# Strassen's scheme for the first matrix of the second network, in a fused linear-attention kernel

## The chip, the cores and the metric

The kernel runs on one core of a Trainium2 chip. The metric is the device time of one execution in microseconds (us): 1276.09 us for the kernel before, the median of 3 runs (1276.03 to 1276.48).

## What is computed

The reference is a linear attention over 8 batches, 8 heads, 576 positions of 64 values, followed by two feed-forward networks over the 4608 tokens of 512 values. All of it is float32. The change touches the second network:

```
def _moe2_ref(x, w_in, w_out, g_ln):        # x 4608x512, w_in 512x1024, w_out 1024x512
    h = x @ w_in
    h_max = np.max(h, axis=-1, keepdims=True)
    e = np.exp(h - h_max)
    sm = e / (np.sum(e, axis=-1, keepdims=True) + 1e-09)
    solu = h * sm
    mu = np.mean(solu, axis=-1, keepdims=True)
    var = np.mean((solu - mu) ** 2, axis=-1, keepdims=True)
    ln = (solu - mu) / np.sqrt(var + 1e-06) * g_ln
    return (ln @ w_out).astype(np.float32)
```

## The kernel before

TensorE (PE) gets its precision from float32r in two parts: each operand x is held as xh, the value rounded by a copy to float32r, and xl = x - xh. A product of two such operands is three matmuls: high by high, high by low, low by high. Each line of matmuls below is such a triple, each matmul 128 rows deep with 512 columns.

The work has two stages. In the **first stage**, nine chunks of 512 tokens go through attention and the first network (`up` into bank pairs `ps_h`, the activation on VectorE and ScalarE, `down` into `ps_y`). A chunk's result goes to DRAM (`y_scratch`) by `y_copy` on ScalarE and `store_y` on SyncE (SP). In chunk 8, `LAST`, the weights of the second network are loaded and split as well. In the **second stage** 36 tiles of 128 tokens go through the second network, four tiles r = 0..3 for each m = 0..8. For one tile:

- `m1_product` (L1315, matmuls L1328, L1329, L1333): 4 parts of the depth of 512 by 2 halves of 1024 columns by 3 matmuls, 24 in all, into one of two bank pairs, `ps_m` for even tiles and `ps_h` for odd ones.
- `softmax_tile` on VectorE (DVE): the maximum (L1104, reads the banks), sum and reciprocal (L1113, L1115), the product `solu` = h x 1/sum x e (L1117, reads the banks and `e2`), the mean (L1120).
- ScalarE (ACT): `exp_tile` (L776, reads the banks), `square_tile` (L783, sums the squares).
- `norm_tile`: the variance on DVE (L1126), the power -1/2 on GpSimd (POOL, L609), then `z` on DVE (L1132), a transpose in blocks of 32 by 32 on DVE (L1138) into `zb`.
- SP stores `zb` to DRAM (`store_z`, L449) and loads it back in four pieces with the blocks in transposed places (`load_z`, L455); ACT and DVE split it into `zh` (L795) and `zl` (L1142).
- `m2_product` (L1402 to L1404): 24 matmuls into `ps_y`; ACT copies the result (L805) and SP stores it (L442).
- The next x tiles are loaded (`load_x2`, L430), copied to their high part on ACT (L811), and the low part is made on POOL (L575).

Every engine has its order written out by hand and runs it strictly in that order; semaphores are the waits. On PE the order is first product of tile r+1, second product of tile r-2:

```
            def tiles(m, first=False, last=False):
                for r in range(4):
                    if not (first and r == 0 or last and r == 3):
                        m1_product(m + (r + 1) // 4, (r + 1) % 4, first=(first and r < 3))
                    if r >= 2:
                        m2_product(m, r - 2, first=first)
                    elif not first:
                        m2_product(m - 1, r + 2)
```

## Time and profile before

| | |
|---|---|
| median of 3 runs | 1276.09 us |
| the profiled execution's own time | 1276.15 us |
| its span in the profile | 1274.3 us |
| PE busy | 1260.3 us, 99% of the span |
| DVE, ACT, POOL busy | 709.6, 387.3, 346.2 us |
| PE's granted clock | 0.997 of full speed |

The span is the time between the first and the last instruction of the profile. Busy is the time in which at least one instruction of that engine ran; a matmul's record is longer than the distance to the next one, since matmuls overlap in the array. So the price of one matmul is read from the distance of two starts, not from its record. Stage two begins at about 875 us.

### The profile page before, as it was taken

Reading aid. Unit: us, or ns where it says so; the run is one execution under the profiler, and the core shown is the slowest. Engines: PE = TensorE matmul, PEld = TensorE weight load, DVE = VectorE, ACT = ScalarE, POOL = GpSimd, SP = SyncE. Lnnn points to the kernel's source line nnn. Section 1 sums busy time; section 2 is a strip of 40 time slices with the busy share of each in tenths; the row PEclk is TensorE's granted clock in tenths of the full one; section 3 lists DMA queues with packets and bytes.
Section 4 is the critical chain, followed back from the end, with each engine's and each line's share of the span. In section 5 each row is a group of like instructions: output and inputs, shape, how many; then the busy total and the mean of one; then the engine's idle time right before and its main releaser. Section 6 shows DMA issues by size and latency. Waiting matters only on the chain.

```text
span 1274.3 us, 16844 instructions
## 1 busy us (share of the span) xinstructions
PE 1260.3 (99%) x6181; PEld 1035.7 (81%) x6181; DVE 709.6 (56%) x989; ACT 387.3 (30%) x625; POOL 346.2 (27%) x289
## 2 busy tenths in 40 slices
PE   7999999999999999999999999999999999999998
PEld 6788887887887887887887888888888888888887
DVE  7865645645645745645745323346755555555553
ACT  4333212212212212212222212124544444444432
POOL 5333233233233233233233222223111111111110
PEclk8999999999999999999999999999999999999999
DMA  8532313313313313313312101210644444444432
GB/s 207 141 120 70 101 38 113 98 37 111 99 37 110 100 37 108 102 37 108 103 37 70 67 1 69 64 67 29 206 155 147 148 142 138 148 147 141 148 124 75
DMA packets 151569, 127.41 MB, mean 100 GB/s; under 512 B 58584, under 2 KB 131824, under 8 KB 150640
## 3 DMA queue, kind: packets, MB, share of 16 engines
q1 hardware_dynamic: 151488, 126.96, 33.0%
q8 instruction: 20, 0.33, 0.1%
q14 instruction: 13, 0.11, 0.0%
q10 hardware_dynamic: 48, 0.01, 0.0%
HBM read 82.33 MB, written 44.61 MB: 100 GB/s over the span
## 4 chain that ended last, share of the span: by engine, by line
PE 97%; DVE 2%; ACT 0%; issue 0%; DMA 0%; POOL 0%; DVEq 0%
PE ps_h L1262 10%; PE ps_h L1264 10%; PE ps_h L1263 10%; PE ps_y L1278 10%; PE ps_y L1279 10%; PE ps_y L1280 10%; PE ps_y L1403 5%; PE ps_y L1404 5%; PE ps_y L1402 5%; PE ps_m L1329 3%; PE ps_h L1329 3%; PE ps_h L1333 3%; PE ps_m L1333 3%; PE ps_h L1328 3%; PE ps_m L1328 3%; PE ps_m L1188 2%
## 5 line engine op out<-in xcount | busy, mean ns | idle before, releaser
L560 POOL TENSOR_TENSOR gl<-tg,gh 128x512 fp32r<-128x512 f32 x144 | 192.7, 1338 | 580.3 <-ACT gh L686 580.3
L686 ACT ACTIVATE gh<-tg 128x512 fp32r<-128x512 f32 x144 | 91.0, 632 | 592.7 <-PE ps_y L1280 427.5
L998 DVE TENSOR_SCALAR tg<-ps_h,acols 128x512 f32<-128x512 f32 x144 | 107.7, 748 | 235.5 <-PE ps_h L1264 233.7
L1262 PE MATMUL ps_h<-xh,W 128*128 128x512 f32 x576 | 227.2, 394 | 0.1
L1264 PE MATMUL ps_h<-xh,W 128*128 128x512 f32 x576 | 224.8, 390 | 0.0
L1263 PE MATMUL ps_h<-xl,W 128*128 128x512 f32 x576 | 224.6, 390 | 0.0
L1278 PE MATMUL ps_y<-gh,WO 128*128 128x512 f32 x576 | 224.6, 390 | 0.0
L1279 PE MATMUL ps_y<-gl,WO 128*128 128x512 f32 x576 | 224.5, 390 | 0.0
L1280 PE MATMUL ps_y<-gh,WO 128*128 128x512 f32 x576 | 224.5, 390 | 0.0
L1262 PEld LDWEIGHTS ps_h<-xh,W 128*128 128x128 f32 x576 | 108.2, 188 | 23.7 <-DVE W L989 0.5
L1264 PEld LDWEIGHTS ps_h<-xh,W 128*128 128x128 f32 x576 | 108.2, 188 | 22.8
L1280 PEld LDWEIGHTS ps_y<-gh,WO 128*128 128x128 f32 x576 | 108.2, 188 | 22.5
L1279 PEld LDWEIGHTS ps_y<-gl,WO 128*128 128x128 f32 x576 | 108.2, 188 | 22.4
L1278 PEld LDWEIGHTS ps_y<-gh,WO 128*128 128x128 f32 x576 | 108.2, 188 | 22.4
L1263 PEld LDWEIGHTS ps_h<-xl,W 128*128 128x128 f32 x576 | 108.3, 188 | 21.7
L1402 PE MATMUL ps_y<-WO,zh 128*128 128x512 f32 x288 | 112.3, 390 | 0.0
L1404 PE MATMUL ps_y<-WO,zl 128*128 128x512 f32 x288 | 112.2, 390 | 0.0
L1403 PE MATMUL ps_y<-WO,zh 128*128 128x512 f32 x288 | 112.2, 390 | 0.0
L1001 DVE SCALAR_TENSOR_TENSOR tg<-ps_h,tg 128x512 f32<-128x512 f32 x144 | 99.6, 692 | 5.0
L1402 PEld LDWEIGHTS ps_y<-WO,zh 128*128 128x128 f32 x288 | 54.1, 188 | 11.2
L1404 PEld LDWEIGHTS ps_y<-WO,zl 128*128 128x128 f32 x288 | 54.1, 188 | 11.1
L1403 PEld LDWEIGHTS ps_y<-WO,zh 128*128 128x128 f32 x288 | 54.1, 188 | 11.1
(166 smaller groups left out, 1633.5 us busy)
## 6 DMA issues: line engine op xcount, KB each, us to landing
z_scratch<-zb SPq DMA_DIRECT2D x35, 512.0 KB, 2.6
zt<-z_scratch SPq DMA_DIRECT2D x140, 128.0 KB, 3.0
y_scratch<-stage SPq DMA_DIRECT2D x36, 256.0 KB, 3.7
A<-k_dram SPq DMA_DIRECT2D x16, 512.0 KB, 4.9
V<-v_dram SPq DMA_DIRECT2D x32, 256.0 KB, 4.7
out_dram<-ost SPq DMA_DIRECT2D x32, 256.0 KB, 2.3
A<-q_dram SPq DMA_DIRECT2D x14, 512.0 KB, 4.9
stage<-kx_scratch SPq DMA_DIRECT2D x6, 1024.0 KB, 4.4
```

The costliest lines, as they stand in the source:

```text
L560: nc.gpsimd.tensor_tensor(gl[:, f % 2, :], tg[:, f % 2, :], gh[:, f % 2, :].bitcast(F32), ALU.subtract).then_inc(gl_ok, 1)
L998: nc.vector.tensor_scalar(tg[:, f % 2, :], ps_h[:, f % 2, :], 0.0, slope[:, f:f + 1], ALU.min, ALU.mult).then_inc(t_ok, 1)
L1001: nc.vector.scalar_tensor_tensor(tg[:, f % 2, :], ps_h[:, f % 2, :], 0.0, tg[:, f % 2, :], ALU.max, ALU.add).then_inc(g_ok, 1)
L1262: nc.tensor.matmul(o, W1[:, f, 0, a, :], xh[:, a, :], start=(a == 0), stop=False)
L1263: nc.tensor.matmul(o, W1[:, f, 0, a, :], xl[:, a, :], start=False, stop=False)
L1264: mm = nc.tensor.matmul(o, W1[:, f, 1, a, :], xh[:, a, :], start=False, stop=(a == KT - 1))
L1278: nc.tensor.matmul(o, WO[:, f, 0, cols], gh[:, f % 2, :], start=(f == 0), stop=False)
L1279: nc.tensor.matmul(o, WO[:, f, 0, cols], gl[:, f % 2, :], start=False, stop=False)
L1280: mm = nc.tensor.matmul(o, WO[:, f, 1, cols], gh[:, f % 2, :], start=False, stop=(f == NF - 1))
L1402: nc.tensor.matmul(o, zh[:, r % 2, f * P:(f + 1) * P], WO2[:, f, 0, :], start=(f == 0), stop=False)
L1403: nc.tensor.matmul(o, zh[:, r % 2, f * P:(f + 1) * P], WO2[:, f, 1, :], start=False, stop=False)
L1404: mm = nc.tensor.matmul(o, zl[:, r % 2, f * P:(f + 1) * P], WO2[:, f, 0, :], start=False, stop=(f == NF2 - 1))
```

## The change

Two tiles of 128 tokens, a **pair**, now go through the first matrix together. A pair is i = 2m + h, 18 of them. The 256 tokens by 512 by 1024 product is cut into two by two blocks and done by seven block products in place of eight (Strassen's scheme, in Winograd's form with few sums). A block product is 2 parts of the depth by 3 matmuls, so 6 matmuls.

- The seven combinations of the weight's blocks are made once, in chunk 8 (`w2_turn` on POOL, `w2_high` on ACT, `w2_low` on DVE). For x, POOL makes four sums of 128x256 a pair (`x2_sums`), ACT copies 128x1024 and 128x768 (`x2_high`), and POOL makes two low parts of these sizes (`x2_low`).
- The seven products go into three banks, `ba` and `bb` (the two of `ps_m`) and `bd` (one of `ps_h`). Block 0 into `ba` is copied out to `p1` by ACT before block 3 adds to the same bank; sums `u1` (before block 4) and `q1` (before block 5) are made by DVE from a bank and `p1`; `c22` is read before block 6. The results c11, c12, c21, c22 are written to `solu` in SBUF, by one ACT copy and three DVE sums. The maximum, `exp` and the product `solu` then read SBUF, no longer the banks.
- `z` moves from DVE to ACT (`norm_tile`, an Identity with scale and bias); its bias is made by a tiny DVE product (`norm_shift`). The variance is a sum scaled by constants, whose factor goes into the gains.
- On PE the order is: seven blocks of pair i, second product of tile 1 of pair i-2, second product of tile 0 of pair i-1. At the start, the blocks of pair 0 stand inside chunk 8 (behind `up` of f = 14), and pair 1 is followed by one second product only. At the end both tiles of pair 17 are transposed by PE (8 transposes each, before: one tile).
- SP's order is, for a pair: output of tile 0 of pair i-2, `store_z` of tile 1 of pair i-1, `load_z` of both tiles of pair i-1, x of pair i+2, output of tile 1 of pair i-2, `store_z` of tile 0 of pair i.

The diff, cut to its core:

```
--- before.py
+++ after.py
-            W2 = sb("W2", [P, 2, KT, F2], F32R)
+            W2c = sb("W2c", [P, 7, 2, 2, TOK], F32R)
             WO2 = sb("WO2", [P, NF2, 2, DM], F32R)
+            solu = sb("solu", [P, 2, F2])
             e2 = sb("e2", [P, 2, F2])
-            solu = sb("solu", [P, 2, F2])
-            junk = sb("junk", [P, F2])
-            z = sb("z", [P, F2])
+            z = sb("z", [P, 2, F2])
             zh = sb("zh", [P, 2, F2], F32R)
             zl = sb("zl", [P, 2, F2], F32R)
-            ost = sb("ost", [P, 2, DM])
...
+            x2raw = sb("x2raw", [P, 2, 2 * TOK])
...
+            xsum = sb("xsum", [P, 3 * 2 * P])
...
+        w2_block = [raw2[a][:, :].rearrange("p (a n) -> p a n", a=2)[:, :, n * TOK:(n + 1) * TOK]
+                    for a in range(2) for n in range(2)]
+        B11, B12, B21, B22 = w2_block
+        w2_part = (B11, B12, B12, B21, B11, B22, B21)
...
+        WO_ORDER = (2, 3, 0, 4, 5, 6, 7, 1)
+        LEFT = (0, 4, 5, 1, 2, 6, 3)
+        p1 = kmax[:, :]
+        u1 = x2b[:, :, :].rearrange("p a n -> p (a n)")
+        q1 = kmt[:, :]
...
+            def pair(m, h, count=2, last=False):
+                before, two_before = ((m - 1, 2), (m - 1, 0)) if h == 0 else ((m, 0), (m - 1, 2))
+                if count >= 2:
+                    store_out(*two_before)
+                if count >= 1:
...
+                    store_z(before[0], before[1] + 1)
...
+                    for t in range(2):
+                        load_z(before[0], before[1] + t)
...
+                if not last:
+                    load_x2(m + 1, h)
+                if count >= 2:
+                    store_out(two_before[0], two_before[1] + 1)
+                if not (last and h == 1):
+                    store_z(m, 2 * h)
...
+            def x2_sums(i, h, m):
+                pool.wait_ge(x2_in[h], 32 * (m + 1))
+                a11, a12, a21, a22 = (x2raw[:, h, n * 2 * P:(n + 1) * 2 * P] for n in range(4))
+                s1, s2, s4 = (xsum[:, n * 2 * P:(n + 1) * 2 * P] for n in range(3))
+                if not (isinstance(i, int) and i == 0):
+                    pool.wait_ge(x2l_ok, 2 * i)
+                nc.gpsimd.tensor_tensor(s1, a21, a22, ALU.add).then_inc(xs_ok, 1)
+                pool.wait_ge(xs_ok, 4 * i + 1)
+                nc.gpsimd.tensor_tensor(s2, s1, a11, ALU.subtract).then_inc(xs_ok, 1)
+                nc.gpsimd.tensor_tensor(a21, a11, a21, ALU.subtract).then_inc(xs_ok, 1)
+                pool.wait_ge(xs_ok, 4 * i + 2)
+                nc.gpsimd.tensor_tensor(s4, a12, s2, ALU.subtract).then_inc(xs_ok, 1)
+            def x2_low(i, h, part):
+                x2h, x2l = x2_parts(i)
+                lo, hi = ((0, 8 * P), (8 * P, 14 * P))[part]
+                src = x2raw[:, h, :] if part == 0 else xsum[:, :]
+                pool.wait_ge(x2h_ok, 2 * i + part + 1)
+                nc.gpsimd.tensor_tensor(x2l[:, lo:hi], src, x2h[:, lo:hi].bitcast(F32),
                                         ALU.subtract).then_inc(x2l_ok, 1)
+            def power(i, t):
+                pool.wait_ge(var_ok, 2 * i + t + 1)
+                nc.gpsimd.tensor_tensor(st[:, t, 8:9], st[:, t, 9:10], mhalf[:, :], ALU.pow).then_inc(rstd_ok, 1)
...
+            for t in range(2):
+                x2_low(1, 1, t)
+            for t in range(2):
+                power(0, t)
+            def pair(m, h, last=False):
+                i = 2 * m + h
+                if not last:
+                    x2_sums(i + 1, 1 - h, m + h)
+                for t in range(2):
+                    if not last:
+                        x2_low(i + 1, 1 - h, t)
+                    power(i, t)
...
+            def p1_copy(i):
+                act.wait_ge(prod, 7 * i + 1)
+                if not (isinstance(i, int) and i == 0):
+                    act.wait_ge(c21_ok, i)
+                nc.scalar.activation(p1, ba, ACT.Copy).then_inc(p1_ok, 1)
+            def c11_copy(i):
+                act.wait_ge(prod, 7 * i + 4)
+                if isinstance(i, int) and i == 0:
+                    act.wait_ge(y_used, NF * LAST + 8)
+                else:
+                    act.wait_ge(z_ok, 2 * i - 1)
+                nc.scalar.activation(solu[:, 0, 0:TOK], ba, ACT.Copy).then_inc(c11_ok, 1)
...
+            def exp_tile(i, t):
+                act.wait_ge(nmax_ok, 2 * i + t + 1)
+                if isinstance(i, int) and i == 0:
+                    act.wait_ge(prod, 7)
+                nc.scalar.activation(e2[:, t, :], solu[:, t, :], ACT.Exp,
+                                     bias=st[:, t, 0:1], accum_out=st[:, t, 1:2]).then_inc(exp_ok, 1)
...
+            def square_tile(i, t):
+                act.wait_ge(nmu_ok, 2 * i + t + 1)
+                if not (isinstance(i, int) and i == 0):
+                    act.wait_ge(zb_ok, 2 * i + t - 1)
+                nc.scalar.activation(z[:, t, :], solu[:, t, :], ACT.Square, bias=st[:, t, 5:6],
+                                     accum_out=st[:, t, 6:7]).then_inc(sq_ok, 1)
+            def norm_tile(i, t):
+                act.wait_ge(nb_ok, 2 * i + t + 1)
+                nc.scalar.activation(z[:, t, :], solu[:, t, :], ACT.Identity, bias=st[:, t, 7:8],
+                                     scale=st[:, t, 8:9]).then_inc(z_ok, 1)
...
+            p1_copy(0)
+            wo2_high(WO_ORDER[2])
+            c11_copy(0)
+            exp_tile(0, 0)
+            x2_high(1, 1)
+            g_high(LAST, NF - 1)
+            exp_tile(0, 1)
+            for f in WO_ORDER[3:]:
+                wo2_high(f)
+            for t in range(2):
+                square_tile(0, t)
+                norm_tile(0, t)
+            y_copy(LAST)
+            def pair(m, h, count=2, last=False):
+                i = 2 * m + h
+                if count >= 2:
+                    out_copy(i - 2, 0)
+                p1_copy(i)
+                c11_copy(i)
+                zt_high(i - 1, 0)
+                exp_tile(i, 0)
+                if not (last and h == 1):
+                    x2_high(i + 1, 1 - h)
+                exp_tile(i, 1)
+                square_tile(i, 0)
+                norm_tile(i, 0)
+                square_tile(i, 1)
+                zt_high(i - 1, 1)
+                norm_tile(i, 1)
+                if count >= 2:
+                    out_copy(i - 2, 1)
...
+            def q1_sum(i):
+                dve.wait_ge(prod, 7 * i + 2)
+                dve.wait_ge(p1_ok, i + 1)
...
+                nc.vector.tensor_tensor(q1, bb, p1, ALU.add).then_inc(q1_ok, 1)
+            def u1_sum(i):
+                dve.wait_ge(prod, 7 * i + 3)
...
+                nc.vector.tensor_tensor(u1, bd, p1, ALU.add).then_inc(u1_ok, 1)
...
+                nc.vector.tensor_tensor(solu[:, 1, TOK:F2], bd, q1, ALU.add).then_inc(c22_ok, 1)
...
+                nc.vector.tensor_tensor(solu[:, 0, TOK:F2], bb, u1, ALU.add).then_inc(c12_ok, 1)
...
+                nc.vector.tensor_tensor(solu[:, 1, 0:TOK], bd, p1, ALU.add).then_inc(c21_ok, 1)
...
+                nc.vector.tensor_reduce(st[:, t, 0:1], solu[:, t, :], AX_X, ALU.max, negate=True).then_inc(nmax_ok, 1)
...
+                nc.vector.scalar_tensor_tensor(solu[:, t, :], solu[:, t, :], st[:, t, 3:4], e2[:, t, :], ALU.mult,
+                                               ALU.mult, accum_out=st[:, t, 4:5]).then_inc(solu_ok, 1)
...
+            def norm_shift(i, t):
+                n = 2 * i + t + 1
+                dve.wait_ge(rstd_ok, n)
+                nc.vector.tensor_tensor(st[:, t, 7:8], st[:, t, 5:6], st[:, t, 8:9], ALU.mult).then_inc(nb_ok, 1)
...
+            def pair(m, h, count=2, last=False):
+                i = 2 * m + h
+                q1_sum(i)
+                u1_sum(i)
+                c22_sum(i)
+                c12_sum(i)
+                max_tile(i, 0)
+                c21_sum(i)
+                max_tile(i, 1)
+                zt_low(i - 1, 0)
+                solu_tile(i, 0)
+                solu_tile(i, 1)
+                norm_stats(i, 0)
+                norm_shift(i, 0)
+                norm_stats(i, 1)
+                zt_low(i - 1, 1)
+                norm_shift(i, 1)
+                if not (last and h == 1):
+                    z_turn(i, 0)
+                    z_turn(i, 1)
...
+                def block(k, bank, more=False):
+                    a = LEFT[k] * 2 * P
+                    if k == 1:
+                        pe.wait_ge(x2l_ok, 2 * i + 2)
+                    if first:
+                        pe.wait_ge(w2_lo, k + 1)
+                    for j in range(2):
+                        hi, lo = (t[:, a + j * P:a + (j + 1) * P] for t in (x2h, x2l))
+                        nc.tensor.matmul(bank, hi, W2c[:, k, 0, j, :], start=(j == 0 and not more), stop=False,
+                                         skip_group_check=more)
+                        nc.tensor.matmul(bank, hi, W2c[:, k, 1, j, :], start=False, stop=False, skip_group_check=more)
+                        mm = nc.tensor.matmul(bank, lo, W2c[:, k, 0, j, :], start=False, stop=(j == 1), skip_group_check=more)
+                    mm.then_inc(prod, 1)
+                if not first:
+                    pe.wait_ge(c11_ok, i)
+                block(0, ba)
+                if not first:
+                    pe.wait_ge(c12_ok, i)
+                block(1, bb)
+                if not first:
+                    pe.wait_ge(c21_ok, i)
+                block(2, bd)
+                pe.wait_ge(p1_ok, i + 1)
+                block(3, ba, more=True)
+                pe.wait_ge(u1_ok, i + 1)
+                block(4, bd, more=True)
+                pe.wait_ge(q1_ok, i + 1)
+                block(5, bb, more=True)
+                pe.wait_ge(c22_ok, i + 1)
+                block(6, bd, more=True)
...
+            def pair(m, h, count=2):
+                i = 2 * m + h
+                m1_pair(i)
+                if count >= 2:
+                    m2_product(i - 2, 1)
+                m2_product(i - 1, 0)
...
+            z_transpose(2 * LAST + 1, 0)
+            m2_product(2 * LAST, 1, turn=True)
+            for t in range(2):
+                m2_product(2 * LAST + 1, t)
```

Where the rows of the order stand now. POOL, for one pair, the last in which x is prepared (`xsum` and `x2raw` hold the sums and the raw x, `st` the statistics). Before, for two tiles:

```order
L575 TENSOR_TENSOR qTl<-V,qTh 128x512 [waits x2h_ok]
L609 TENSOR_TENSOR st<-st,mhalf 128x1 [waits var_ok]
L575 TENSOR_TENSOR qTl<-A,qTh 128x512 [waits x2h_ok]
L609 TENSOR_TENSOR st<-st,mhalf 128x1 [waits var_ok]
L575 TENSOR_TENSOR qTl<-kmax,qTh 128x512 [waits x2h_ok]
```

Now, for one pair:

```order
L608 TENSOR_TENSOR xsum<-x2raw 128x256 [waits x2l_ok,x2_in1]
L610 TENSOR_TENSOR xsum<-xsum,x2raw 128x256 [waits xs_ok]
L611 TENSOR_TENSOR x2raw<-x2raw 128x256
L613 TENSOR_TENSOR xsum<-x2raw,xsum 128x256 [waits xs_ok]
L620 TENSOR_TENSOR xl<-x2raw,xh 128x1024 [waits x2h_ok]
L625 TENSOR_TENSOR st<-st,mhalf 128x1 [waits var_ok]
L620 TENSOR_TENSOR xl<-xsum,xh 128x768 [waits x2h_ok]
```

The second low part stands directly behind the power of tile 0. The power of tile 1 follows it, and the sums for the next pair stand directly behind that one.

DVE, from `solu` to the end of a tile. Before (the `z` row is the one that goes to ACT):

```order
L1142 TENSOR_TENSOR zl<-zt,zh 128x1024 [waits zh_ok]
L1113 TENSOR_SCALAR st<-st 128x1 [waits exp_ok]
L1115 RECIPROCAL st<-st 128x1 [waits se_ok]
L1117 SCALAR_TENSOR_TENSOR solu,st<-ps_h,st,e 128x1024 [waits rs_ok]
L1120 TENSOR_SCALAR st<-st 128x1 [waits solu_ok]
L1126 TENSOR_SCALAR st<-st 128x1 [waits sq_ok]
L1132 TENSOR_SCALAR z<-solu,st 128x1024 [waits zb_ok,rstd_ok]
L1138 STREAM_TRANSPOSE zb<-z 128x1024 [waits zb_st,z_ok]
```

Now, for the two tiles of a pair, behind the maxima and the low part of tile 0 of the pair before:

```order
L1279 RECIPROCAL st<-st 128x1 [waits se_ok]
L1281 SCALAR_TENSOR_TENSOR solu,st<-solu,st,e 128x1024 [waits rs_ok]
L1284 TENSOR_SCALAR st<-st 128x1 [waits solu_ok]
L1277 TENSOR_SCALAR st<-st 128x1 [waits exp_ok]
L1279 RECIPROCAL st<-st 128x1 [waits se_ok]
L1281 SCALAR_TENSOR_TENSOR solu,st<-solu,st,e 128x1024 [waits rs_ok]
L1284 TENSOR_SCALAR st<-st 128x1 [waits solu_ok]
L1289 TENSOR_SCALAR st<-st 128x1 [waits sq_ok]
L1294 TENSOR_TENSOR st<-st 128x1 [waits rstd_ok]
L1289 TENSOR_SCALAR st<-st 128x1 [waits sq_ok]
L1308 TENSOR_TENSOR zl<-A,zh 128x1024 [waits m2_done,zh_ok]
L1294 TENSOR_TENSOR st<-st 128x1 [waits rstd_ok]
```

L1281 reads `solu` and `e`, both in SBUF, where L1117 read a bank and `e`. L1294 is the new tiny product (`norm_shift`), and the low part of tile 1 of the pair before stands ahead of its second instance. Both transposes follow.

ACT, for one pair (`tg` is the output buffer, `kmax` is `p1`, `A` is `zt`):

```order
L898 ACTIVATE tg<-ps_y 128x512 [waits o_st0,m2_done]
L850 ACTIVATE kmax<-ps_m 128x512 [waits c21_ok,prod]
L858 ACTIVATE solu<-ps_m 128x512 [waits z_ok,prod]
L889 ACTIVATE zh<-A 128x1024 [waits m2_done,zt_in0]
L864 ACTIVATE e,st<-solu,st 128x1024 [waits nmax_ok]
L912 ACTIVATE xh<-x2raw 128x1024 [waits prod,xs_ok]
L912 ACTIVATE xh<-xsum 128x768
L864 ACTIVATE e,st<-solu,st 128x1024 [waits nmax_ok]
L871 ACTIVATE z,st<-solu,st 128x1024 [waits zb_ok,nmu_ok]
L876 ACTIVATE z<-solu,st 128x1024 [waits nb_ok]
L871 ACTIVATE z,st<-solu,st 128x1024 [waits zb_ok,nmu_ok]
L889 ACTIVATE zh<-A 128x1024 [waits m2_done,zt_in1]
```

Behind them come `z` of tile 1 (L876) and the output of tile 1 of pair i-2, and then the next pair's L898 and L850. The copy to `p1` (L850), for which PE waits, thus stands behind all of the pair before.

## Rows read from the trace of the kernel before

**Rows 1.** The page: busy time, and the chain that ended last, by engine.

```profile
PE 1260.3 (99%) x6181; PEld 1035.7 (81%) x6181; DVE 709.6 (56%) x989; ACT 387.3 (30%) x625; POOL 346.2 (27%) x289
...
PE 97%; DVE 2%; ACT 0%; issue 0%; DMA 0%; POOL 0%; DVEq 0%
```

**Rows 2.** Waits of PE: what it waited for, total, times, longest.

```profile
PE ps_m L1163 <- DVE kmax L883: 3.1, 2, 1.7
```

**Rows 3.** Timeline of PE in stage two: start, length, instruction.

```profile
1062.59 0.39 PE L1402 MATMUL ps_y<-WO,zh 128*128 128x512 f32 x1
...
1068.03 0.39 PE L1328 MATMUL ps_h<-W,qTh 128*128 128x512 f32 x1
```

**Rows 4.** Instructions by line and form: busy us, mean ns, idle before.

```profile
L560 POOL TENSOR_TENSOR gl<-tg,gh 128x512 fp32r<-128x512 f32 x144 | 192.7, 1338 | 580.3 <-ACT gh L686 580.3
...
L1142 DVE TENSOR_TENSOR zl<-zt,zh 128x1024 fp32r<-128x1024 f32 x35 | 42.5, 1215 | 0.0
L783 ACT ACTIVATE junk<-solu,st 128x1024 f32<-128x1024 f32 x36 | 41.5, 1153 | 51.2 <-DVE st L1120 51.2
L795 ACT ACTIVATE zh<-zt 128x1024 fp32r<-128x1024 f32 x35 | 37.0, 1057 | 6.6 <-DMA zt<-z_scratch 6.4
...
L1117 DVE SCALAR_TENSOR_TENSOR solu<-ps_m,st,e 128x1024 f32<-128x1024 f32 x18 | 23.1, 1284 | 0.6
...
L1104 DVE TENSOR_REDUCE st<-ps_m 128x1 f32<-128x1024 f32 x18 | 22.0, 1220 | 34.1 <-PE ps_m L1333 34.1
...
L805 ACT ACTIVATE ost<-ps_y 128x512 f32<-128x512 f32 x36 | 21.5, 599 | 15.9 <-PE ps_y L1404 12.9 <-ACT junk L783 1.1
...
L985 DVE TENSOR_TENSOR xl<-ps_m,xh 128x512 fp32r<-128x512 f32 x28 | 19.4, 692 | 45.4 <-ACT xh L675 45.4
```

**Rows 5.** Timeline of one tile in stage two, all engines.

```profile
1062.79 1.22 DVE L1104 TENSOR_REDUCE st<-ps_m 128x1 f32<-128x1024 f32 x1 [2.20 <-PE ps_m L1333]
...
1064.05 1.12 ACT L776 ACTIVATE e<-ps_m,st 128x1024 f32<-128x1024 f32 x1 [4.83 <-DVE st L1104]
...
1065.15 0.62 ACT L811 ACTIVATE qTh<-kmax 128x512 fp32r<-128x512 f32 x1
...
1068.70 0.55 POOL L609 TENSOR_TENSOR st<-st,mhalf 128x1 f32<-128x1 f32 x1 [1.55 <-DVE st L1126]
```

**Rows 6.** Timeline: the way of the first tile's z through DRAM.

```profile
887.73 0.34 SPq L449 DMA_DIRECT2D z_scratch<-zb  x1
890.39 1.75 SPq L455 DMA_DIRECT2D zt<-z_scratch  x4
...
894.94 1.06 ACT L795 ACTIVATE zh<-zt 128x1024 fp32r<-128x1024 f32 x1 [1.23 <-DMA zt<-z_scratch]
```

**Rows 7.** Timeline: DVE beside POOL, in chunk 8 and behind it.

```profile
856.84 1.29 POOL L560 TENSOR_TENSOR gl<-tg,gh 128x512 fp32r<-128x512 f32 x1 [4.15 <-ACT gh L686]
857.41 1.26 DVE L1084 SCALAR_TENSOR_TENSOR WO<-V,acols,WO 128x512 fp32r<-128x512 f32 x1 [2.25 <-ACT WO L818]
...
880.94 0.75 DVE L1084 SCALAR_TENSOR_TENSOR WO<-A,acols,WO 128x512 fp32r<-128x512 f32 x1 [1.88 <-ACT WO L818]
881.51 1.34 POOL L575 TENSOR_TENSOR qTl<-V,qTh 128x512 fp32r<-128x512 f32 x1 [6.60 <-ACT qTh L811]
...
881.99 1.28 DVE L1117 SCALAR_TENSOR_TENSOR solu<-ps_m,st,e 128x1024 f32<-128x1024 f32 x1
```

**Rows 8.** The same at the start of the kernel, POOL's row and DVE's.

```profile
10.82 1.04 POOL L538 TENSOR_TENSOR qTh<-ident,km 128x512 fp32r<-128x512 f32 x1 [8.13 <-DVE km L906]
...
10.91 0.97 DVE L911 TENSOR_TENSOR kml<-km,kmh 128x4 f32<-128x4 f32 x1
```

**Rows 9.** Stretches: busy time of PE, PEld, DVE, ACT, POOL, clock, DMA.

```profile
9.00:12.00 3.00, 0.74 (x5) 0.51 (x5) 2.90 (x7) 0.00 (x0) 1.08 (x2) 0.88 1.31 262
12.00:15.00 3.00, 2.66 (x9) 2.06 (x10) 3.00 (x4) 0.87 (x2) 3.00 (x3) 0.50 1.37 217
...
18.00:21.00 3.00, 3.00 (x63) 2.54 (x64) 2.71 (x5) 2.30 (x3) 2.37 (x2) 0.99 0.28 87
```

560 lines of the change are left out of this document (289 added, 271 removed).

## The prediction

> **What bounds the kernel now.** The page comes first: PE is busy 99% of the span and is 97% of the chain that ended last [rows 1]. The list of PE's waits is next: its largest entry is 3.1 us at the start of the kernel, and nothing in it belongs to stage two [rows 2]. So in stage two PE streams without a gap, and every other engine has slack. The price of a matmul comes from the distance of starts: the 24 matmuls of one second product run from 1062.59 to 1068.03, which is 5.44 us, or 0.2267 us each [rows 3]. Two tiles take 96 matmuls, 21.76 us. The groups by line then give the price of each step on the other engines [rows 4], and the timeline of one tile gives their order and the hand-over times [rows 5]. These steps form a long chain (maximum, exponential, solu, square, power, z, transpose, DRAM, split), but today PE has a first and a second product between any two of its uses, so the chain is never seen.
>
> **Fewer matmuls.** A pair has 7 x 6 = 42 matmuls in place of 48. 18 pairs save 108, and 108 x 0.2267 = 24.5 us. All of it lies on PE, which sets the end. A pair now asks 42 + 48 = 90 matmuls of PE, 20.40 us.
>
> **The new loop.** This gain holds only if PE need not wait. Before, PE's only conditions in stage two were results a tile old or older. Now block 3 waits for `p1`, a copy of block 0 of the same pair. That copy stands on ACT behind all of the pair before, down to its last `z` and two output copies; and that pair's chain starts at its own blocks 3 to 5, which it needs for c12. So the time from one block 3 to the next is at least the length of this loop. I add it up with the rows' durations; an ACT instruction directly behind another costs about 0.1 less than its record (1064.05 to 1065.15 for a record of 1.12), and a hand-over costs 0.04 (the maximum ends at 1064.01, ACT starts at 1064.05) [rows 5].
>
> - Blocks 3, 4, 5: 18 matmuls, 4.08; until DVE starts 0.20 (PE's next product starts at 1062.59, DVE at 1062.79) [rows 3, 5]. At 4.28.
> - c12, a sum of a bank and SBUF, as L985: 0.73. Maximum over 1024, as L1104: 1.25 [rows 4]. At 6.26.
> - The exponential stands on ACT behind `zh` of the pair before, which waits for DRAM. From the issue of the store to that of the load are 2.66, from there to the start of `zh` 4.55 [rows 6]. The store of tile 0 stands on SP behind the output of tile 1 of an older pair, and goes at 24.4 of the loop before; `zh` starts at 6.6 of this one and takes 0.96, so the exponential waits to 7.53.
> - Exponential 1.15; x's high parts, 1024 and 768 wide, 0.96 + 0.71 (1.05 for 1024, 0.62 for 512 [rows 4, 5]); second exponential 1.28; two tiny ones 0.36. At 11.98.
> - `solu` of tile 1: 1.29 as L1117, and 0.84 held up by POOL (below). Mean and variance 0.34, hand-over 0.08, power 0.55 [rows 5]. At 15.1.
> - `norm_shift` 0.19, and 1.60 held up by POOL. `z` on ACT: I take the square's 1.15, less 0.1, as it has the same width and also a bias [rows 4]. At 17.9.
> - Square of tile 1 1.15, `zh` of tile 1 1.09, `zl` 1.22 and 0.33 held up, `norm_shift` 0.10 and 0.50 held up, `z` 1.10. At 23.4.
> - Two output copies 0.51 each and the copy to `p1` 0.64 (L805 [rows 4]). At 25.0.
>
> 25.0 against 20.4 of PE work leaves PE idle for 4.6 us in each pair. What is late next is block 1 of the next pair, for its second low part, by under 0.1. Pair 2 starts from a disturbed order and I take 5 for it, 5.2 for pair 3, 13 x 4.6 = 60 for pairs 4 to 16, and 3.8 for pair 17, behind which POOL has less work. Together 74 us.
>
> **The port.** The largest new term is where POOL holds DVE up. A DVE instruction with two inputs in SBUF took 1.26 us when it started 0.57 behind a POOL one, and 0.75 with POOL idle; the one that reads a bank and SBUF took 1.28 beside POOL, its usual time [rows 7, 4]. Size does not help: a product of 128x4 that started 0.09 behind a POOL instruction of 1.04 ended with it, after 0.97 [rows 8]. `solu` moves from the harmless kind to the other, and `norm_shift` is of that kind. POOL has four sums (0.73 each), two low parts (2.41 and 1.85) and two powers in each pair, estimated from L560's 1.29 at 512 wide and a slope of 2.2 ns per column. Its second low part starts directly behind the power, the very instruction `norm_shift` waits for, so it holds that one up for 1.6 in every pair. These hold-ups are 0.84 + 1.60 + 0.33 + 0.50 = 3.3 us of the loop. Bounds: 0 if DVE always got there first, 4.3 if the first `solu` met the first low part too.
>
> At `norm_shift` the two starts lie within 0.1 us, and a tie could also go DVE's way (third rival). The Trainium skill (SBUF — State Buffer, "Who interferes with whom") has this as a rule against such a change: two SBUF inputs of DVE and a reading GpSimd instruction share one read interface, and the second to issue blocks until the first is done, whatever its size. By it the sum is the forecast's; without it, the second rival's.
>
> **The start of stage two.** In chunk 8 DVE is 1.3 late for the sum before block 4 of pair 0. From the end of pair 0's blocks, PE has 48 matmuls of chunk 8 and three blocks of pair 1, 15.0 us. ACT has in front of `p1` of pair 1: two exponentials, x's high parts, a `g_high`, five copies of weights, both squares and both `z`, and then the four copies of `y_copy`. The squares and `z` wait for DVE, whose five low parts of weights meet POOL's 2.41 and 1.85. Followed in this way it comes to 25.5 us, so 10.1 is wait, and 0.4 is for a low part of x. The first second product then waits 3.8 for its z from DRAM, and pair 2 1.1 for x. Together 16.7 us. Bounds: 10, if DVE and POOL don't meet, and 20.
>
> **The end.** Pair 17 is short of cover: the second product of pair 16 waits for the output copy that stands behind the last `z`, 2.9, and there are 8 more transposes, 0.9. Together 3.8.
>
> **Work with no price.** The seven weight combinations (14 instructions of DVE and ACT, four of POOL) lie in chunk 8, where PE has 24 matmuls, 5.44 us, for each step f, and POOL one L560 [rows 3, 4]. If that cover were gone, they would cost about 1.2 each on DVE (L1142's width). The x loads are two transfers per pair, two pairs ahead. SP's queue is charged above, with the store and the load.
>
> **The sum.** 1276.15 - 24.5 + 74 + 16.7 + 3.8 = 1346.2 us, from the profiled execution's own time, which is 0.06 above the median. My forecast is **1346 us**, slower.
>
> **Rivals.**
> 1. **The clock falls in PE's gaps: 1370 us.** From 9 to 12 us PE was busy for only 0.74, the clock granted was 0.88 in that stretch and 0.50, the lower of the two levels (1.2 GHz), behind it, and 0.99 again from 18 on [rows 9]. A gap of 4.6 in each pair is of that size. At half speed for 2 to 5 us a pair loses 1 to 2.5; 16 pairs at 1.5 are 24 us. Against it: PE works 20 us between two gaps here. The Trainium skill (TensorE: Matmul & The Clock Gate, "Why this matters for your kernels") warns of idle gaps between bursts of matmuls, and by it the fall would come.
> 2. **The loop without the port: 1296 us.** If hand-overs fall so that POOL never holds DVE, the loop is 25.0 - 3.3 = 21.7, idle 1.3 in 16 pairs, 21 us; start 13, end 3, and 7 for DRAM traffic in bursts (two stores and two outputs go out together now). 1276 - 24.5 + 44 = 1296.
> 3. **Only `norm_shift` gets through: 1316 us.** Loop 23.1, idle 2.7, 43 us; start and end 18; traffic 3: 1276 - 24.5 + 64 = 1316. For it: the power's result and the low part's start are under 0.1 apart.
> 4. **Faster, 1262 us.** The loop is shorter than PE's 20.4 us: without the port, and the DRAM way at least 1.3 shorter than now, as one transfer is no longer behind another. Then only the start is paid: 1276 - 24.5 + 10. Its point is a loop of 20.4; by the rows the loop without port and DRAM is still 20.4 to 20.6.
>
> That the change does not do what it says can be left out: the 108 matmuls are gone from the order.
>
> **How the numbers follow.** Forecast 0.42, clock 0.20, third rival 0.15, loop without the port 0.11, faster 0.08, no change 0.04. A measurement of this kernel tells 0.2% (2.6 us) from no change. The forecast's own range is 1332 to 1358: 0.8 either way per pair. The whole range runs from 1292, which takes in the rival without the port, to 1386, the clock falling in nearly every pair; about 0.18 lies outside. Faster 0.08, same 0.04, slower 0.88.
>
> **What would show it.** Right: PE waits for ACT's copy to `p1` 17 times, some 4.6 us each and once about 10; starts of block 0 are 25 us apart; `norm_shift` has a median near 1.7 us for a 128x1 product, and `solu` of one of two tiles lies over 2 us; stage-two PE busy near 82%. Wrong: `norm_shift` at 0.15 (third rival); `solu` at 1.3 too (second); a granted clock under 0.95 behind the gaps (first); PE without waits for `p1` (fourth).

## The result, and the profile after

The changed kernel takes **1386.8 us**, the median of 4 runs (1386.1 to 1388.0), against 1276.08 for the kernel before: a ratio of 1.0867, 95% interval 1.0854 to 1.0881. It is slower, as forecast, but by 110.7 us where 70 were forecast, and 0.8 us above the top of the range. The page of the profile after opens with these rows (busy time of each engine, and the chain that ended last by engine and by line):

```profile
PE 1273.9 (92%) x6081; PEld 1035.7 (75%) x6081; DVE 813.5 (59%) x1084; ACT 459.3 (33%) x700; POOL 453.4 (33%) x363
...
issue 15%; POOL 6%; DVE 5%; PE 4%; ACT 4%; DMA 3%; SPq 0%; POOLq 0%; ACTq 0%; DVEq 0%
POOL xl L620 4%; DVE st L1294 2%; DMA A<-z_scratch 1%; DMA z_scratch<-V 1%; DVE solu L1281 1%; ACT z L871 1%; POOL xsum L610 1%; POOL st L625 1%; ACT zh L889 1%; PE ps_m L1533 1%; ACT e L864 1%; DVE WO L1214 1%; PE ps_m L1536 0%; PE ps_m L1535 0%; ACT xh L912 0%
```

PE was 97% of this chain before [rows 1]; now a mixture of every engine stands there, with POOL's low parts (`xl`, L620) as its first line. (The shares add up to 37%, as the chain is followed back only to about 870 us; "issue" is time in which the profile shows no wait.) PE's waits name the place (what PE waited for, us in total, times, the longest):

```profile
PE ps_m L1533 <- ACT kmax L850: 87.7, 17, 9.1
PE ps_y L1630 <- DVE zl L1308: 3.7, 1, 3.7
...
PE ps_y L1630 <- ACT tg L898: 2.9, 1, 2.9
```

L850 is the copy to `p1` (its buffer is called `kmax`). It is waited for 17 times, 87.7 us in all, one of them 9.1 at the start: the wait that was forecast, where it was forecast, and nearly as long (84 us in the forecast). Nothing of the kind stood in the list before [rows 2].

One wait, in the timeline of PE (start, duration, engine, line, output and inputs, form, idle time before and its releaser):

```profile
1062.64 0.39 PE L1536 MATMUL ps_h<-W2c,xl 128*128 128x512 f32 x1
1068.15 0.80 PE L1533 MATMUL ps_m<-W2c,xh 128*128 128x512 f32 x1 [5.12 <-ACT kmax L850]
1068.74 0.63 PE L1535 MATMUL ps_m<-W2c,xh 128*128 128x512 f32 x1
1069.17 0.63 PE L1536 MATMUL ps_m<-W2c,xl 128*128 128x512 f32 x1
1069.60 0.63 PE L1533 MATMUL ps_m<-W2c,xh 128*128 128x512 f32 x1
...
1072.07 0.39 PE L1535 MATMUL ps_h<-W2c,xh 128*128 128x512 f32 x1
1072.30 0.39 PE L1536 MATMUL ps_h<-W2c,xl 128*128 128x512 f32 x1
```

After 5.1 us of idling the matmuls start 0.427 us apart, twice the 0.227 of [rows 3], and only from about 1071.6 on 0.227 again. The next block 3 starts at 1095.33, so a pair takes 27.18 us here. The other engines' timeline in the same pair:

```profile
1075.67 1.06 ACT L889 ACTIVATE zh<-A 128x1024 fp32r<-128x1024 f32 x1 [3.87 <-DMA A<-z_scratch]
1076.63 1.14 ACT L864 ACTIVATE e<-solu,st 128x1024 f32<-128x1024 f32 x1
...
1079.38 3.05 DVE L1281 SCALAR_TENSOR_TENSOR solu<-solu,st,e 128x1024 f32<-128x1024 f32 x1
1082.96 1.29 DVE L1281 SCALAR_TENSOR_TENSOR solu<-solu,st,e 128x1024 f32<-128x1024 f32 x1
1085.16 1.78 DVE L1294 TENSOR_TENSOR st<-st 128x1 f32<-128x1 f32 x1 [0.66 <-POOL st L625]
...
1078.89 2.46 POOL L620 TENSOR_TENSOR xl<-x2raw,xh 128x1024 fp32r<-128x1024 f32 x1 [12.16 <-ACT xh L912]
1085.10 1.84 POOL L620 TENSOR_TENSOR xl<-xsum,xh 128x768 fp32r<-128x768 f32 x1
```

The `solu` of tile 0 starts 0.49 behind POOL's first low part and takes 3.05; that of tile 1, with POOL idle, takes 1.29. `norm_shift` (L1294), one number a row, takes 1.78 and ends with POOL's second low part.

### The profile page after: what moved, and what is told of

It reads as the page before. It is cut to its first block and busy times, and to the rows that moved or that the text cites. A ratio compares the mean times of both kernels' runs of the same rounds, so it can differ in the third digit from the quotient of the medians.

```text
span 1385.0 us, 17034 instructions
## 1 busy us (share of the span) xinstructions
PE 1273.9 (92%) x6081; PEld 1035.7 (75%) x6081; DVE 813.5 (59%) x1084; ACT 459.3 (33%) x700; POOL 453.4 (33%) x363
## 5 line engine op out<-in xcount | busy, mean ns | idle before, releaser
L1533 PE MATMUL ps_m<-W2c,xh 128*128 128x512 f32 x136 | 63.1, 464 | 88.4 <-ACT kmax L850 87.7
L1467 PEld LDWEIGHTS ps_h<-xh,W 128*128 128x128 f32 x576 | 108.1, 188 | 23.8 <-DVE W L1111 0.5
L1483 PEld LDWEIGHTS ps_y<-gh,WO 128*128 128x128 f32 x576 | 108.1, 188 | 22.9 <-POOL gl L589 0.4
L1469 PEld LDWEIGHTS ps_h<-xh,W 128*128 128x128 f32 x576 | 108.1, 188 | 22.8
L620 POOL TENSOR_TENSOR xl<-x2raw,xh 128x1024 fp32r<-128x1024 f32 x17 | 45.3, 2665 | 196.4 <-ACT xh L912 196.4
L1533 PEld LDWEIGHTS ps_m<-W2c,xh 128*128 128x128 f32 x136 | 29.0, 214 | 101.9 <-ACT kmax L850 94.8
```

The costliest lines, as they stand in the source:

```text
L1467: nc.tensor.matmul(o, W1[:, f, 0, a, :], xh[:, a, :], start=(a == 0), stop=False)
L1469: mm = nc.tensor.matmul(o, W1[:, f, 1, a, :], xh[:, a, :], start=False, stop=(a == KT - 1))
L1483: nc.tensor.matmul(o, WO[:, f, 0, cols], gh[:, f % 2, :], start=(f == 0), stop=False)
L1533: nc.tensor.matmul(bank, hi, W2c[:, k, 0, j, :], start=(j == 0 and not more), stop=False, skip_group_check=more)
```

## The experiments

Three causes are to be told apart: **the port** (POOL's large instructions hold DVE up), **the clock** (it falls in PE's gaps), and **the order** (what ACT's order puts in a row makes the loop, and places POOL's work against DVE's). "Period" below is the distance of two copies to `p1` (or of two c11 copies), averaged over 11 to 13 pairs in the middle of stage two; for the change it is 27.4 us. Ratios are to the kernel before, with 95% intervals.

| kernel | us | ratio | period |
|---|---|---|---|
| the change | 1386.8 | 1.0867 [1.0854, 1.0881] | 27.4 |
| a1 norm_shift, one tensor input | 1348.0 | 1.0567 [1.0550, 1.0585] | 24.3 |
| a2 12 filling matmuls | 1384.0 | 1.0846 [1.0828, 1.0864] | 27.2 |
| b3 20 filling matmuls | 1365.4 | 1.0693 [1.0675, 1.0710] | 25.9 |
| a3 a1 and 12 filling matmuls | 1334.6 | 1.0462 [1.0444, 1.0479] | 23.8 |
| a4 POOL's work 8 columns wide | 1315.8 | 1.0308 [1.0291, 1.0326] | 22.8 |
| b1 z back on VectorE | 1320.2 | 1.0346 [1.0328, 1.0363] | 23.9 |
| c3 ACT's order, first half | 1383.9 | 1.0841 [1.0824, 1.0858] | 27.3 |
| c2 ACT's order, second half | 1363.0 | 1.0677 [1.0661, 1.0694] | 25.9 |
| b2 ACT's order, both halves | 1287.7 | 1.0086 [1.0070, 1.0103] | 21.3 |
| b4 b2 and a1 | 1278.0 | 1.0012 [1.0002, 1.0021] | 20.7 |
| c4 b1 and b2 | 1295.1 | 1.0150 [1.0135, 1.0166] | 22.1 |
| c1 b4 and another start | 1270.3 | 0.9956 [0.9943, 0.9970] | 20.7 |

**a1: one operand of `norm_shift` in another form.**

```
-                nc.vector.tensor_tensor(st[:, t, 7:8], st[:, t, 5:6], st[:, t, 8:9], ALU.mult)
+                nc.vector.tensor_scalar(st[:, t, 7:8], st[:, t, 5:6], st[:, t, 8:9], None, ALU.mult)
```

> One instruction in another form: norm_shift takes the power's result as its per-partition scalar and no longer as a second tensor, so it has one tensor input in SBUF; the number is the same. Theory A (POOL's second low part holds norm_shift up, 1.6 to 1.8 us for tile 1 and 0.5 for tile 0 in each pair, both on the loop from block 3 to block 3): norm_shift falls from 1.78 to about 0.15, the period from 27.2 to about 24.4 us, the time to about 1336 us. Rival B (norm_shift is long because POOL's power hands its result over late, whatever the form): it stays at 1.7 and the time at 1387. Rival C (the length of the order alone, with the DRAM way as its longest piece, sets the period): norm_shift is short, the time goes down by under 10 us.

Measured: 1348.0 us (1343.9 to 1350.1), period 24.3. (In the expectation the tiles are swapped: it is tile 0's `norm_shift` that takes 1.78, tile 1's takes 0.67.) Groups by line of DVE from 940 to 1240 us (busy us, mean ns of one, idle before), the change first and then a1:

```profile
L1281 DVE SCALAR_TENSOR_TENSOR solu<-solu,st,e 128x1024 f32<-128x1024 f32 x22 | 47.6, 2166 | 0.8
L1308 DVE TENSOR_TENSOR zl<-A,zh 128x1024 fp32r<-128x1024 f32 x22 | 31.0, 1409 | 8.8 <-ACT zh L889 8.8
L1294 DVE TENSOR_TENSOR st<-st 128x1 f32<-128x1 f32 x22 | 27.1, 1231 | 7.3 <-POOL st L625 7.3
```

```profile
L1281 DVE SCALAR_TENSOR_TENSOR solu<-solu,st,e 128x1024 f32<-128x1024 f32 x26 | 46.6, 1791 | 0.9
...
L1294 DVE TENSOR_SCALAR st<-st 128x1 f32<-128x1 f32 x24 | 5.0, 208 | 7.9 <-POOL st L625 7.9
```

The same product of 128x1, at the same place and behind the same power, takes 0.21 us in place of 1.23 on average. All that changed is how the second operand is given, so it was not the power's result that came late (rival B falls). The form of a product of one number a row is worth 39 us; a part of that lies in `solu`, whose mean also fell, from 2.17 to 1.79, as the starts on DVE and POOL moved.

The time is still 12 us above the 1336 expected. PE's gaps are now 2.2 to 3.3 us long, and behind 7 of the 16 the clock falls again (spacing 0.43), as at 1056.70, behind a gap of 2.9. Behind the other 9 it does not, though one of them is the longest of all:

```profile
1129.78 0.50 PE L1533 MATMUL ps_m<-W2c,xh 128*128 128x512 f32 x1 [3.29 <-ACT kmax L850]
1130.11 0.39 PE L1535 MATMUL ps_m<-W2c,xh 128*128 128x512 f32 x1
1130.34 0.40 PE L1536 MATMUL ps_m<-W2c,xl 128*128 128x512 f32 x1
```

A pair with a fall takes 25.0 to 26.5 us, one without 23.6 to 24.2, so seven falls cost some 13 us, about what is missing. (This is the execution of 1343.9 us; the other three have a lower clock and take longer.)

**a2 and b3: filling matmuls in PE's gap.** They write a bank that nothing reads.

```
                 block(2, bd)
+                for _ in range(0 if first else 12):
+                    nc.tensor.matmul(ps_h[:, 1, :], x2h[:, 0:P], W2c[:, 0, 0, 0, :], start=True, stop=True)
                 pe.wait_ge(p1_ok, i + 1)
```

> 12 matmuls of 512 columns that write an unused bank stand on PE between block 2 and the wait for p1, in pairs 1 to 17; they bring PE's granted clock through the gap and compute nothing that is read. Theory A (in the gap of 5.1 us the clock falls, and the first blocks behind it run at half speed for 1.6 us): the period goes from 27.2 to about 25.6, the time to 1355 to 1362 us, and the spacing behind the wait stays 0.227. Rival B (the fall is hidden, as the loop waits for DVE and ACT anyway): within 3 us of 1387. Rival C (the filling delays the real blocks): slower than 1387 by up to 10.

> 20 filling matmuls (4.5 us) in place of 12 between block 2 and the wait for p1. With 12 a gap of 2.4 us was left in each pair, and the clock fell behind it all the same. Theory A (a fall costs about 1.6 us a pair, and it comes with gaps of over 2 us, not with those under 1): no spacing over 0.23 us behind the wait, period 25.8, time 1360 to 1364. Rival B (the clock is no term of the loop): 1384 as with 12. Rival C (the filling delays block 3): slower than 1384.

Measured: 1384.0 with 12, only 3 us less; 1365.4 with 20, 21.5 us less. The timeline of PE with 12, then (in the second fence) the only gap with 20 from 1056 to 1084 us:

```profile
1064.41 0.79 PE L1533 MATMUL ps_m<-W2c,xh 128*128 128x512 f32 x1 [2.39 <-ACT kmax L850]
1065.00 0.63 PE L1535 MATMUL ps_m<-W2c,xh 128*128 128x512 f32 x1
1065.43 0.63 PE L1536 MATMUL ps_m<-W2c,xl 128*128 128x512 f32 x1
```

```profile
1063.28 0.50 PE L1533 MATMUL ps_m<-W2c,xh 128*128 128x512 f32 x1 [0.73 <-ACT kmax L850]
```

And the stretch from 925 to 1250 us (length, busy us of PE, PEld, DVE, ACT, POOL with counts, granted clock, DMA share, GB/s), of the change, with 12 and with 20:

```profile
925.00:1250.00 325.00, 265.40 (x1068) 213.90 (x1067) 222.34 (x300) 151.58 (x212) 109.49 (x96) 0.92 0.40 115
```

```profile
925.00:1250.00 325.00, 298.16 (x1235) 240.76 (x1234) 221.09 (x301) 154.40 (x217) 112.10 (x97) 0.95 0.40 115
```

```profile
925.00:1250.00 325.00, 317.09 (x1381) 257.54 (x1380) 220.86 (x310) 157.63 (x223) 119.89 (x101) 1.00 0.42 122
```

My expectation for 12 was wrong: I took it that a gap of about 2.4 us would leave the clock alone, and behind 12 gaps of 2.3 to 2.6 us in a row it fell to the lower level (behind the two before them, of 2.07 and 2.63, it did not). With 20, the gap is 0.7, the clock stays at 1.00, and the period goes down by 1.5 us, the price of the slow first blocks: (0.427 - 0.227) x 8 = 1.6. The clock is a term of the loop of its own, worth 21.5 us, and the filling cost nothing that shows.

**a3: both.** 

> Both edits, norm_shift with one tensor input and the 12 filling matmuls. If port and clock are separate terms, their gains add up but for the shorter gap, which leaves the clock less to lose: about 1324 us, period 23.7. If the two are one and the same cause (the gap is only long because of the port), it is the time of the first edit alone, 1336.

Measured: 1334.6, against 1324 expected. The number alone would fit the rival's 1336, but that was the time expected of a1, and a1 took 1348.0: the filling gives 13.4 us on top of it, where it gave 3 without a1. So the two are separate terms. The granted clock is 1.00 and the waits for `p1` are down to 10.2 us in all, so now the filling sets the period: 90 + 12 matmuls at 0.2267 are 23.1 us of the 23.8.

**a4: POOL's sums and low parts of x 8 columns wide.**

```
+                if not (isinstance(i, int) and i < 2):
+                    a11, a12, a21, a22, s1, s2, s4 = (v[:, 0:8] for v in (a11, a12, a21, a22, s1, s2, s4))
...
+                if not (isinstance(i, int) and i < 2):
+                    src, hi = src[:, 0:8], lo + 8
```

> From pair 2 on POOL's four sums of x and its two low parts are only 8 columns wide in place of 256, 1024 and 768: the combinations and low parts of x are left out but for these columns, and the output is not the reference's. The filling is not in. Theory A (POOL's large instructions hold up solu, zl and norm_shift, together about 4.2 us of the loop): all three fall to their undisturbed times (1.29, 1.22, 0.15), the period to about 23.1 us, the time to about 1314. If only norm_shift is held in a way that counts, it is the time of the first kernel of this set, about 1336. If POOL has no part in it, 1387.

```profile
L1285 DVE SCALAR_TENSOR_TENSOR solu<-solu,st,e 128x1024 f32<-128x1024 f32 x27 | 34.7, 1286 | 0.9
L1312 DVE TENSOR_TENSOR zl<-A,zh 128x1024 fp32r<-128x1024 f32 x26 | 31.8, 1224 | 14.4 <-ACT zh L893 14.3
L1298 DVE TENSOR_TENSOR st<-st 128x1 f32<-128x1 f32 x27 | 4.3, 159 | 9.2 <-POOL st L629 9.2
```

Measured: 1315.8, 2 us from the 1314 expected (the output is not the reference's, as most of x's sums and low parts are left out). `solu`, `zl` and `norm_shift`, in their old forms, all fall to their undisturbed 1.29, 1.22 and 0.16. So every one of these hold-ups is POOL's work, and together (with the clock that a shorter gap loses less of) they are 71 of the 111 us. That POOL's own results now come sooner is no part of it for the two powers: in the change POOL stood idle for 3.24 and 2.69 us ahead of them.

**b1: z back on VectorE.** This undoes one part of the change.

```
             def norm_tile(i, t):
-                act.wait_ge(nb_ok, 2 * i + t + 1)
-                nc.scalar.activation(z[:, t, :], solu[:, t, :], ACT.Identity, bias=st[:, t, 7:8],
-                                     scale=st[:, t, 8:9]).then_inc(z_ok, 1)
+                pass
...
-                nc.vector.tensor_tensor(st[:, t, 7:8], st[:, t, 5:6], st[:, t, 8:9], ALU.mult).then_inc(nb_ok, 1)
+                nc.vector.tensor_scalar(z[:, t, :], solu[:, t, :], st[:, t, 5:6], st[:, t, 8:9], ALU.add,
+                                        ALU.mult).then_inc(z_ok, 1)
```

> One part of the change undone: z is made on VectorE again, in one instruction as in the kernel before (0.81 us there), at the place where norm_shift stood; norm_shift and ScalarE's two z are gone. Theory A (the loop is a sum of steps on two engines, and z on ScalarE with its tiny bias product costs norm_shift 1.78 + 1.24 against 0.81 for tile 0, 0.67 + 1.24 against 0.81 for tile 1, and delays ScalarE's squares and copies): the period falls from 27.4 to about 21.6 us and the time to about 1286 us, range 1278 to 1310. Rival B (VectorE becomes the bound, as it has the most work beside TensorE): period about 25, time about 1345. Rival C (the new z, with one tensor input in SBUF, is held up by POOL as norm_shift was): z on VectorE takes over 2 us for tile 0 and the time is about 1310 to 1330.

Measured: 1320.2. Theory A had the direction, rival C the reason why it is not 1286. The timeline of DVE, then of POOL:

```profile
1057.21 2.33 DVE L1292 TENSOR_SCALAR z<-solu,st 128x1024 f32<-128x1024 f32 x1 [0.66 <-POOL st L625]
...
1061.18 1.21 DVE L1292 TENSOR_SCALAR z<-solu,st 128x1024 f32<-128x1024 f32 x1 [0.45 <-POOL st L625]
```

```profile
1057.14 1.85 POOL L620 TENSOR_TENSOR xl<-xsum,xh 128x768 fp32r<-128x768 f32 x1
```

z, with one tensor in SBUF, took 0.81 us before and takes 2.33 when it starts 0.07 behind a low part. The end is 0.55 behind POOL's. The Trainium skill (SBUF — State Buffer, "Who interferes with whom") names this case too: a `tensor_scalar` that runs in a mode with two ports takes the pair that GpSimd uses. The trace agrees in that z is held, and that alone, at 0.81 us, it is faster than the other DVE instructions of 1024 columns (1.2 to 1.3); in which mode it ran no run shows. The 128x1 product of a1, of the same kind of instruction, was not held.

**b2, c3, c2: ACT's order.** No instruction is added or taken away. The whole of b2:

```
                 p1_copy(i)
                 c11_copy(i)
+                x2_high(i + 1, 1 - h, parts=(0,))
                 zt_high(i - 1, 0)
                 exp_tile(i, 0)
-                x2_high(i + 1, 1 - h)
                 exp_tile(i, 1)
+                x2_high(i + 1, 1 - h, parts=(1,))
                 square_tile(i, 0)
-                norm_tile(i, 0)
-                square_tile(i, 1)
                 zt_high(i - 1, 1)
-                norm_tile(i, 1)
+                square_tile(i, 1)
+                norm_tile(i, 0)
                 out_copy(i - 2, 1)
+                norm_tile(i, 1)
```

> The order of ScalarE's instructions in a pair alone is changed: x's first high part stands before zh of tile 0 (it fills the wait for DRAM), the second exponential before x's second high part, zh of tile 1 and both squares before the z of tile 0, and the second output copy before the z of tile 1. No instruction is added or taken away. Theory A (the loop is made of what the order puts in a row, and the hold-up of solu and norm_shift by POOL comes from the moments at which the order lets POOL's low parts start): period about 21.2 us, time about 1285, range 1276 to 1320. Rival B (POOL's instructions hold VectorE up wherever they stand, and the sum of steps is the same): within 15 us of 1387. Rival C: only the hand-over of the exponential gets shorter, about 1377.

> Only the first half of ScalarE's new order: x's first high part ahead of zh of tile 0, the second exponential ahead of x's second high part. Theory A (the time saved ahead of the second exponential is given back, as tile 0's norm_shift and z, and behind them the square of tile 1, set the loop): period 27.3, time about 1384, range 1372 to 1388; alone it is worth almost nothing, and it pays only together with the second half. Rival (the halves add up): about 1332, what the full order gained less the second half's gain.

> Of ScalarE's new order only the second half, norm_shift in its old form: both squares, z of tile 0, zh of tile 1, the second output copy, z of tile 1; the first half (zh, exponential, x's high parts, exponential) as in the change. Theory A (the loop's largest piece is that the square of tile 1 stands behind the z of tile 0, which stands behind the held-up norm_shift; with the square ahead, the hold-up and the square run side by side): period about 24.5 us, time about 1340, range 1325 to 1360. Rival (only the first half, in which x's high part fills the DRAM wait, counts): within 5 us of 1387.

Measured: 1287.7 for both halves, 99 us less than the change and 3 from what was expected; 1383.9 for the first half alone, as expected; 1363.0 for the second, above the range I gave. Groups by line of b2, from 940 to 1240 us:

```profile
L1312 DVE TENSOR_TENSOR zl<-A,zh 128x1024 fp32r<-128x1024 f32 x28 | 47.7, 1705 | 0.1
L1285 DVE SCALAR_TENSOR_TENSOR solu<-solu,st,e 128x1024 f32<-128x1024 f32 x30 | 38.6, 1285 | 1.0
L1298 DVE TENSOR_TENSOR st<-st 128x1 f32<-128x1 f32 x28 | 34.8, 1243 | 15.5 <-POOL st L625 15.5
```

`norm_shift` is still held up, 1.24 on average as in the change, and `zl` more than there (1.71 against 1.41), but `solu` no longer: POOL's first low part now starts with x's first high part, ahead of the exponential, and meets `zl` instead. Worked out from these averages and the undisturbed times of a4, the hold-ups of a pair add up to 3.1 us, against 4.3 in the change. So rival B, that hold-ups follow wherever POOL's work stands, is right that most of them stay and wrong about their price. What the order changed is what stands behind them. In the change tile 1's square, `zh`, `zl`, `norm_shift` and z all stand behind the z of tile 0, and that behind the held-up `norm_shift`; from the z of tile 0 to that of tile 1 are 5.6 us (1086.98 to 1092.58). In b2, ACT:

```profile
1070.30 1.04 ACT L889 ACTIVATE zh<-A 128x1024 fp32r<-128x1024 f32 x1
1071.25 1.14 ACT L871 ACTIVATE z<-solu,st 128x1024 f32<-128x1024 f32 x1
...
1073.50 1.25 ACT L876 ACTIVATE z<-solu,st 128x1024 f32<-128x1024 f32 x1 [1.03 <-DVE st L1298]
1074.65 0.58 ACT L898 ACTIVATE tg<-ps_y 128x512 f32<-128x512 f32 x1
1075.83 1.25 ACT L876 ACTIVATE z<-solu,st 128x1024 f32<-128x1024 f32 x1 [0.60 <-DVE st L1298]
```

Now `zh` and the square of tile 1 run while `norm_shift` is held, and the two z are 2.3 us apart. From the copy of c11 to the next copy to `p1` the change takes 23.5 us, b2 18.9 (1058.58 to 1077.45). The clock has a part in this too: of the 5.9 us by which a pair is shorter (27.18 to 21.30), 1.4 lie between block 3 and the sum c12 (5.93 to 4.55), where the matmuls no longer run at the lower level, and 4.5 behind c12.

The halves do not add up: 2.9 and 23.8 us alone, 99 together. In c3 `solu` is free but `zl` ahead of it held (2.2 us), and the square of tile 0 starts 11.6 us behind the copy of c11, in the change 11.5. This looks as if nothing was won, but it is the clock that takes it back. The gap of 4.21 us is followed by 11 matmuls at the lower level, where the change has 6 to 9. PE's block 3 and DVE's sum c12 in c3, and the same sum in the change (its block 3 starts at 1068.15):

```profile
1064.71 0.79 PE L1537 MATMUL ps_m<-W2c,xh 128*128 128x512 f32 x1 [4.21 <-ACT kmax L850]
...
1071.55 0.69 DVE L1263 TENSOR_TENSOR solu<-ps_m,x2b 128x512 f32<-128x512 f32 x1 [0.60 <-PE ps_m L1540]
```

```profile
1074.08 0.69 DVE L1259 TENSOR_TENSOR solu<-ps_m,x2b 128x512 f32<-128x512 f32 x1 [0.57 <-PE ps_m L1536]
```

From block 3 to c12 are 6.84 us in c3 and 5.93 in the change; from c12 to the square 7.81 and 8.58. So the order gained 0.8 us a pair and the clock took 0.9. That c3 came out at the 1384 expected is in this sense luck: I had put it down to the steps behind. Why the clock stayed low for longer is open.

In c2 the first `solu` still takes 3.05 us; the gap left is 3.5 us, and the clock still falls behind it (granted 0.92 over the middle, where b2 has 1.00). That is the larger part of my miss: behind such a gap 5 to 13 matmuls of a pair run at the lower level, at 0.2 us each, which b2 with gaps of 0.5 does not pay.

All this can be added up on PE, over stage two of one execution each (the second row is an estimate from the traces: by how much the starts of matmuls with no wait between them lie further apart than 0.227 us):

| us | the change | c3 | c2 | b2 |
|---|---|---|---|---|
| PE's waits | 96 | 82 | 69 | 22 |
| matmuls at the lower clock | 34 | 45 | 37 | 9 |

Of the 99 us of b2, 74 are waits and 25 the clock. The waits go down by 14 and 27 with the halves alone, so they do not add up either; but c3 loses 11 of its 14 to the clock, and only b2's gaps are short enough to be rid of the falls.

**b4 and c4: with `norm_shift`'s new form, and with z on VectorE.**

> The order of ScalarE as above and norm_shift with one tensor input. Theory A (the two gains overlap, as the floor of TensorE's own 20.4 us a pair is reached): period 20.4, TensorE without waits from pair 4 on, time about 1274, range 1268 to 1290. If the order alone gives nothing: 1348, as with norm_shift alone.

> z on VectorE together with ScalarE's new order (squares, zh and output copy in the same places, no z among them). z on VectorE took 2.33 us beside POOL's low part and 1.21 beside its sums, against 0.81 in the kernel before. Theory A (it is held up by POOL as norm_shift was, in this order too): period about 22, time about 1292, range 1283 to 1302, so z on ScalarE is right once the order is. Rival (in the new order POOL's low part no longer meets z): 0.81 us each, period 20.8, time about 1276.

Measured: 1278.0 and 1295.1, both in their ranges. In b4 PE has no wait from 925 us on, and the period is 20.67 us against 20.40 of matmuls; most of the rest is two starts a pair that come some 0.1 late. In c4 z takes 1.78 us on average and costs 7.4 us against b2, 0.8 in each pair less some 5 that the start gains (PE's wait for `p1` there is 4.3 in place of 9.1): z on ScalarE is the better place once the order is right, though b1 shows it to be the worse one in the change's own order (by 67 us).

**c1: another start.**

```
-            for t in range(2):
-                square_tile(0, t)
-                norm_tile(0, t)
-            y_copy(LAST)
+            for t in range(2):
+                square_tile(0, t)
+            norm_tile(0, 0)
+            p1_copy(1)
+            norm_tile(0, 1)
+            y_copy(LAST)
...
             solu_tile(0, 0)
-            for n in range(3, NF2):
-                wo2_low(n)
             solu_tile(0, 1)
+            wo2_low(3)
+            norm_stats(0, 0)
...
```

(on POOL also the first power ahead of x's second low part)

> On top of ScalarE's new order and norm_shift with one tensor input, the start of stage two is put in another order: on ScalarE both squares of pair 0, then z of tile 0, then the copy to p1 of pair 1, then z of tile 1 and y_copy; on VectorE solu of tile 1 ahead of the five low parts of weights, and the steps of norm between them; on POOL the first power ahead of the second low part of x. Theory (in the start PE waits 8.7 us for p1 and 4.7 for z, and both hang on VectorE's low parts of weights, held up to 6.5 us for four beside POOL, and on y_copy standing ahead of p1): the wait for p1 goes nearly wholly, that for z stays about 4; 1278 less 9.5 is about 1268 us, range 1263 to 1275, faster than the kernel before. Rival (the start is bound by the way of z through DRAM, whatever the order): the wait moves to the first second product and the time stays within 3 us of 1278.

PE's waits in b4 and then in c1:

```profile
PE ps_m L1537 <- ACT kmax L850: 8.7, 1, 8.7
PE ps_y L1634 <- DVE zl L1312: 4.7, 1, 4.7
```

```profile
PE ps_y L1640 <- DVE zl L1313: 4.7, 1, 4.7
...
PE ps_m L1543 <- POOL xl L620: 2.2, 2, 1.9
```

Measured: 1270.3 us (1270.0 to 1271.5). The wait of 8.7 is gone, 1.5 of it came back as a wait for x's low part. This version beats the kernel before, by 0.44% (interval 0.30 to 0.57%), with the same 6081 matmuls as the change: 24.5 us fewer of them, of which the start, with 8 us of waits and the lower clock behind them, takes most back.

## Why the prediction was wrong

The direction, the port and the place of the wait were right. What failed is one term that the sum left out and one that it had too small. **The clock** stood in the sum at nothing, as a rival with a chance of 0.20: it is worth 21.5 us (b3), and in the loop it adds 1.65 us to the 25.0. **The hold-up of the first `solu`** was charged with 0.84 us, for the other tile; it was 1.76, which makes the loop 1.0 longer. PE's waits were forecast at 93.6 us (74, 16.7 and 2.9) and came to 96.1; nearly all of the 40 us that are missing to 1386.8 stand on PE as matmuls at the lower clock (34 us by the estimate above). **Point by point**:

- *Fewer matmuls, -24.5 us*: the spacing is 0.227 wherever the clock is full. c1 shows that the gain is there, once nothing stands in its way.
- *PE waits for `p1` in every pair*: 17 waits, as said; starts 27.2 to 27.8 us apart (the last 26.3) where I said 25.0.
- *The loop, 25.0 us*. Against the pair from 1068.15 to 1095.33 (27.18 us): blocks 3 to 5 took 1.65 more (5.93 from block 3 to the sum c12), all of it clock. The wait for DRAM cost 0.5 of the path, as the maximum ended at 1076.10 and the exponential started at 1076.63; I had 1.27, so 0.74 less. Up to the `norm_shift` of tile 0 the first `solu` adds 1.0. The two z took 1.24 where I took the square's 1.15, 0.2 together. 25.0 + 1.65 - 0.74 + 1.0 + 0.2 is 27.1; the last 0.1 are hand-overs. The gap is 5.1 in place of 4.6, and the rest of the difference is the clock.
- *The port, 3.3 of the loop*: `norm_shift` 1.78 and 0.67 against 0.15 free (I had 1.60 and 0.50 more than that, right, but the median of 1.7 that I named as a sign is 0.67, since only one of the two tiles is held for long), `zl` 1.60 (0.33 more had been taken, it was 0.38). **The step that was mis-sized is `solu`**: I let the `solu` of tile 1 meet the first low part, with 0.84 held; it was the `solu` of tile 0, held for 1.76, and tile 1's stands behind it. I had this as the upper bound, "if the first `solu` met the first low part too". x's first high part stands on ACT directly behind the first exponential, and POOL's low part starts at 1078.89; `solu` stands on DVE behind the other maximum and `zl` and starts at 1079.38, 0.49 too late. Which of the two comes first hung on steps I had worked out to within 0.5 us only.
- *The start, 16.7 us*: the waits are 1.1, 0.7, 9.1 and 3.7, 14.6 in all against 1.3, 0.4, 10.1 and 3.8, and the 1.1 for x in pair 2 did not come; *the end*: the wait for the output copy 2.9, as said. From 875 to 925 us the clock was 0.86, which I had not charged.
- *The first rival, the clock, chance 0.20*: **this is the step that failed.** It should have been in the forecast. b3 measures it at 21.5 us; I had worked out 24. Its mark, the granted clock below 0.95 behind the gaps, is in the trace. I had set against it that PE works 20 us between two gaps; behind none of the change's gaps, 4.0 to 5.2 us in the loop, did this help, and behind shorter ones in other runs not always (see the end). With the clock in the forecast, and `solu` at its bound, the sum is 1346 + 21.5 + 16 x 0.9 = 1382. That this is so near is in part luck, as it keeps the 0.74 a pair too much for DRAM, 12 us in 16 pairs, and has no clock in the start. The sign "stage-two PE busy near 82%" came true by luck as well: it is 265.4 of 325 us, 82%, in a longer loop, since slow matmuls count as busy for longer.
- *The second rival, the loop without the port, 1296*: a4 removes it from pair 2 on and gives 1315.8. The rival left out the clock, which in a4 still falls behind 5 of the 15 gaps in the loop, had the start cheaper, and had the loop at 21.7 where it is 22.8, and mostly 22.4 to 22.9 without a fall: with the hold-ups gone the wait for DRAM grows to 1.66 (in a4 the maximum ends at 1094.79, the exponential starts at 1096.45). Its 7 us for DRAM traffic, and the third rival's 3, no run shows. *The third, 1316*: `norm_shift` alone free gives 1348 (a1), since the first `solu` stays held in part and the clock still falls.
- *The fourth, faster*: its point was a loop of 20.4 us, and I had said that by the rows the loop without port and DRAM is still 20.4 to 20.6. For the change's own order no run comes below that (22.8 in a4, which still has the wait for DRAM). What I had not thought of is that the order was free: the same instructions, with ACT's in another order, make a loop that PE's 20.4 nearly hides.

## What to carry to other kernels

When a chain of steps becomes a loop, price it twice: the sum of its steps, and each place where another engine's long instruction can meet one of them; the hold-up was nearly as long as the rest of that instruction here, however small the step. Then ask what stands behind the held instruction on its engine, and whether it has to: here the kernel is 99 us faster with x's high part ahead of the wait for DRAM and the square, the split and the output copy ahead of the waiting z, though three quarters of the hold-ups are still there. And a gap on PE is not priced at its length alone: look in the trace for what the clock does behind gaps of that size, in many pairs and not in one, before it is put down as a rival. When an edit gains nothing, see whether the clock has taken the gain back, as in c3.

## What the runs showed that I had not expected

- A gap of 2.39 us on PE, behind over 20 us of work without a pause, was followed by seven matmuls at the lower clock level (spacing 0.427 us). The length of the gap alone does not tell whether the clock falls. From pair 2 on none of the gaps of up to 1.75 us in any run was followed by a fall (0.5 in b2, 0.7 in b3, 1.4 in c4); of those from 1.9 to 3.3 us some were and some were not, and the longest of a1, 3.29, was not; all from 3.35 us up were. What decides in between no run shows. In c2, where the gap is 3.5 us, the clock in several pairs fell only when PE had started again, in one 1.3 us after it, at 1060.28 (spacing 0.23 to 1061.32, 0.43 from 1061.58 on).
- The form of the operand decides: a 128x1 product of two SBUF tensors was held for 1.6 us, the same product with one of them given as a scalar per partition took 0.21. But a 128x1024 `tensor_scalar` of that kind was held too (2.33 for 0.81), and beside POOL's sums it took 1.21.
- POOL is held up as well: its sum of 128x256 takes 1.58 us beside DVE's `zl` and 0.72 alone, and its first low part 2.94 in place of 2.41 in c2.
- Matmuls that fill a gap and write an unused bank paid for themselves: 20 a pair, 340 more in all, and the kernel is 21.5 us faster than without them.
